# Weight slices and the first x tile of the feed-forward part: loaded from scan step 31 on, split at steps 33 to 46 in other raw places, ten slices ahead in place of nine

## The reference

```python
# attention, per head: k_n = k / (|k| + 1e-6), head_dim 48
for t in range(S):
    y[:, :, t] = q[:, :, t] @ state
    v_old = state applied to k_n[t]
    state = state + beta[t] * outer(k_n[t], v[t] - v_old)
x = y as (3072, 384)
# feed-forward 1 (d_ff 2048)
h = x @ w_in
g = (a0 + a1*h + a2*h^2 + a3*h^3) / (1 + |b0|*|h| + |b1|*h^2 + 1e-6)
x = g @ w_out
# feed-forward 2 (d_ff 2048)
x = relu(x @ w_in2)^2 @ w_out2
```

## Time and profile before

| | |
|---|---|
| time, median of 3 runs | 1114.39 us (1114.38 to 1116.54) |
| time of the profiled execution | 1114.34 us, span 1112.6 us |
| PE busy | 1094.1 us (98%) |
| DVE, ACT, POOL busy | 678.0 (61%), 650.8 (58%), 509.2 us (46%) |
| chain that ended last | PE 89%, DVE 6%, issue 2%, DMA 1%, POOL 1% |
| granted clock, mean of the span | 0.994 of 2.4 GHz |

### The profile page before, as it was taken

How to read it: one execution, slowest core, us unless ns; L and a number is a source line. 1 busy time by engine, 2 the same in 40 slices (tenths; PEclk the granted TensorE clock), 3 DMA queues, 4 the chain that set the end, 5 groups by cost and what they waited for, 6 DMA issues and landing times.

```text
span 1112.6 us, 18161 instructions
## 1 busy us (share of the span) xinstructions
PE 1094.1 (98%) x6372; PEld 944.5 (85%) x6372; DVE 678.0 (61%) x1088; ACT 650.8 (58%) x1275; POOL 509.2 (46%) x626
## 2 busy tenths in 40 slices
PE   8899999999999999999999999999999999999998
PEld 6699999999987788888888888888888888888887
DVE  6987564434559989787888879854333333434332
ACT  5566666544669777787877778653333323333322
POOL 5087888783039977887777878500000000000000
PEclk9799999999999999999999999999999999999999
DMA  8948887555531110100101002140100101010000
GB/s 193 204 84 182 165 180 151 117 94 149 135 107 57 44 57 1 32 27 1 57 1 57 1 22 93 43 128 1 57 1 9 49 1 57 0 57 1 1 29 29
DMA packets 173658, 74.41 MB, mean 67 GB/s; under 512 B 136000, under 2 KB 161728, under 8 KB 172608
## 3 DMA queue, kind: packets, MB, share of 16 engines
q1 hardware_dynamic: 163968, 68.54, 25.6%
q10 hardware_dynamic: 9600, 4.72, 1.7%
HBM read 52.27 MB, written 20.71 MB: 66 GB/s over the span
## 4 chain that ended last, share of the span: by engine, by line
PE 89%; DVE 6%; issue 2%; DMA 1%; POOL 1%; SPq 1%; ACT 0%; POOLq 0%; DVEq 0%; ACTq 0%
PE ps L1137 11%; PE ps L1139 11%; PE ps L1138 11%; PE ps L1123 11%; PE ps L1125 11%; PE ps L1124 11%; PE ps L505 3%; PE ps L484 3%; PE ps L549 3%; PE ps L535 3%; PE ps L552 3%; PE ps L515 3%; PE ps L521 2%; PE ps L467 1%; PE ps L563 1%
## 5 line engine op out<-in xcount | busy, mean ns | idle before, releaser
L1123 PE MATMUL ps<-x_split,weights 128*128 128x512 f32 x576 | 225.0, 391 | 3.8 <-DVE g_lo L1282 2.9
L1137 PE MATMUL ps<-g_hi,weights 128*128 128x512 f32 x576 | 224.1, 389 | 0.1
L1124 PE MATMUL ps<-x_split,weights 128*128 128x512 f32 x576 | 224.1, 389 | 0.0
L1125 PE MATMUL ps<-x_split,weights 128*128 128x512 f32 x576 | 224.1, 389 | 0.0
L1138 PE MATMUL ps<-g_lo,weights 128*128 128x512 f32 x576 | 224.1, 389 | 0.0
L1139 PE MATMUL ps<-g_hi,weights 128*128 128x512 f32 x576 | 224.1, 389 | 0.0
L1292 DVE TENSOR_TENSOR common<-common 128x512 f32<-128x512 f32 x96 | 66.4, 691 | 135.0 <-ACT common L1196 133.4
L1202 ACT ACTIVATE g_hi<-common 128x512 fp32r<-128x512 f32 x96 | 60.8, 633 | 141.8 <-PE ps L1139 137.3
L1123 PEld LDWEIGHTS ps<-x_split,weights 128*128 128x128 f32 x576 | 108.1, 188 | 27.9 <-DVE g_lo L1282 4.6
L1341 POOL TENSOR_SCALAR common<-common,b_abs 128x512 f32<-128x512 f32 x96 | 75.8, 789 | 116.1 <-ACT common L1171 116.1
L1355 POOL TENSOR_TENSOR common<-common,g_hi 128x512 f32<-128x512 f32 x96 | 124.4, 1296 | 9.5 <-DVE g_hi L1270 9.5
(11 more groups left out here) (121 smaller groups left out, 1917.4 us busy)
## 6 DMA issues: line engine op xcount, KB each, us to landing
scan_late<-kq_in SPq DMA_DIRECT2D x10, 768.0 KB, 5.4
scan_late<-kq_in SPq DMA_DIRECT2D x16, 384.0 KB, 4.7
shared<-w_in SPq DMA_DIRECT2D x32, 192.0 KB, 2.5
shared<-w_out SPq DMA_DIRECT2D x32, 192.0 KB, 2.6
x_first<-y_t ACTq DMA_DIRECT2D x24, 192.0 KB, 2.9
shared<-x_first SPq DMA_DIRECT2D x6, 768.0 KB, 5.8
x_second<-shared SPq DMA_DIRECT2D x6, 768.0 KB, 4.2
shared<-x_second SPq DMA_DIRECT2D x6, 768.0 KB, 5.9
```

The lines of the kernel that those rows point to most:

```text
L1123: pe.matmul(bank(n), lo, x_hi[:, slot, k, :], start=(k == 0), stop=False)
L1124: pe.matmul(bank(n), hi, x_lo[:, slot, k, :], start=False, stop=False)
L1125: mm = pe.matmul(bank(n), hi, x_hi[:, slot, k, :], start=False, stop=(k == KT - 1))
L1137: pe.matmul(ps_y[m], lo, g_hi[:, d, :], start=(f == 0), stop=False)
```

## The change

Loads and splits get tables of their own by step, and the raw places are taken in another order: slices 0 and 1 go to places 0 and 1, slices 2 and 3 to the same two places again, slices 4 and 5 to places 2 and 3, and from slice 6 on the places go round as before. A slice waits for the split of the slice that had its place (2 for 0, 3 for 1, none for 4 and 5, i-4 from 6 on).

| scan step | before: loads | before: splits | after: loads | after: splits |
|---|---|---|---|---|
| 31, 32 | | | ab and 0; 1 | |
| 33, 34 | | | x | 0; 1 |
| 35, 36 | | | 2; 3 | 2 (step 36) |
| 37 | ab, 0, x, 1, 2, 3 | | 4, 5 | 3 |
| 38 to 40 | 4, 5 (39, 40) | 0 (40) | 6, 7 (39) | x in three pieces |
| 41 to 46 | 6 to 11 | 1 to 6, x at 41, 43, 45 | 8 to 12 (42 to 46) | 4 to 9 |
| 47, 48 | 12 (47) | 7, 8 | 13 (47) | |

```diff
-    FF_LOADS, FF_SPLIT, FF_X = GROUPS - 11, GROUPS - 8, (41, 43, 45)
+    W_LOADS = {31: (0,), 32: (1,), 35: (2,), 36: (3,), 37: (4, 5), 39: (6, 7), 42: (8,), 43: (9,), 44: (10,), 45: (11,),
+               46: (12,), 47: (13,)}
+    W_SPLITS = {33: 0, 34: 1, 36: 2, 37: 3, 41: 4, 42: 5, 43: 6, 44: 7, 45: 8, 46: 9}
+    X_LOAD, X_SPLITS = 33, (38, 39, 40)
...
-                if n == FF_LOADS:
+                if n == min(W_LOADS):
                     ff.load_ab(sp)
-                    ff.load_weights(sp, 0)
+                for i in W_LOADS.get(n, ()):
+                    ff.load_weights(sp, i)
+                if n == X_LOAD:
                     ff.load_x(sp, 0)
-                    for i in range(1, ff.W_SLOTS):
-                        ff.load_weights(sp, i)
-                if 0 <= n - FF_LOADS - 2 < ff.PRE:
-                    ff.load_weights(sp, n - FF_LOADS - 2 + ff.W_SLOTS)
...
-                if 0 <= n - FF_SPLIT < ff.PRE:
-                    ff.split_weights_hi(act, n - FF_SPLIT)
+                if n in W_SPLITS:
+                    ff.split_weights_hi(act, W_SPLITS[n])
...
-    W_SLOTS, W_AHEAD, PRE = 4, 3, 9
+    W_SLOTS, W_AHEAD, PRE = 4, 3, 10
...
+    def raw_slot(i):
+        return i if i < 2 else (i + 2) % W_SLOTS
+
+    def raw_former(i):
+        return {2: 0, 3: 1}.get(i, i - W_SLOTS if i >= 6 else None)
+
+    def raw_loads(i):
+        return 1 if i < 2 else (i + 2) // W_SLOTS + (raw_slot(i) < 2)
...
-        if i >= W_SLOTS:
-            sp.wait_ge(w_lo_ready, i - W_SLOTS + 1)
+        if raw_former(i) is not None:
+            sp.wait_ge(w_lo_ready, raw_former(i) + 1)
...
-        act.wait_ge(w_loaded[i % W_SLOTS], 32 * (i // W_SLOTS) + 32)
+        act.wait_ge(w_loaded[raw_slot(i)], 32 * raw_loads(i))
```

More of the change, by code:

```diff
@@ L739, in _ @@
                     take_z_first(n)
-                if n in FF_X:
-                    ff.split_x_hi(act, FF_X.index(n), 0)
+                if n in X_SPLITS:
+                    ff.split_x_hi(act, X_SPLITS.index(n), 0)
                 spread = (n + 1 + LEAD) // 2 if n > TWICE[1] and n % 2 == 1 and end_group(n + 1) is not None else None
@@ L962, in _ @@
                         scale_v(h)
-                if n == FF_SPLIT:
+                if n == min(W_SPLITS):
                     ff.coef_bounds(dve)
[L965 to L968, removed]
+                if n in W_SPLITS:
+                    ff.split_weights_lo(dve, W_SPLITS[n])
+                if n in X_SPLITS:
+                    ff.split_x_lo(dve, X_SPLITS.index(n), 0)
             ff.vector(dve, ys_done, GROUPS)
@@ L1058, in load_weights @@
     def load_weights(sp, i):
-        m, f, slot = i // FT, i % FT, i % W_SLOTS
-        if i >= W_SLOTS:
-            sp.wait_ge(w_lo_ready, i - W_SLOTS + 1)
+        m, f, slot = i // FT, i % FT, raw_slot(i)
+        if raw_former(i) is not None:
+            sp.wait_ge(w_lo_ready, raw_former(i) + 1)
         sp.dma_start(w_raw[:, slot, 0:D_MODEL].rearrange("p (k n) -> p k n", k=KT),
@@ L1159, in split_weights_hi @@
             act.wait_ge(down_done, UNITS - FT + f + 1)
-        act.activation(weights[:, f, 0:2 * D_MODEL], w_raw[:, i % W_SLOTS], ACT.Copy).then_inc(w_hi_ready, 1)
+        act.activation(weights[:, f, 0:2 * D_MODEL], w_raw[:, raw_slot(i)], ACT.Copy).then_inc(w_hi_ready, 1)
     def split_x_hi(act, k, tile):
@@ L1246, in split_weights_lo @@
         dve.wait_ge(w_hi_ready, i + 1)
-        dve.tensor_tensor(weights[:, f, 2 * D_MODEL:4 * D_MODEL], w_raw[:, i % W_SLOTS],
+        dve.tensor_tensor(weights[:, f, 2 * D_MODEL:4 * D_MODEL], w_raw[:, raw_slot(i)],
                           weights[:, f, 0:2 * D_MODEL].bitcast(F32), ALU.subtract).then_inc(w_lo_ready, 1)
```

## The result

| | before | after |
|---|---|---|
| median, same chip, 17 runs each | 1114.68 us (1113.06 to 1117.54) | 1118.41 us (1115.89 to 1120.67) |
| ratio, 95% interval | | 1.0032 [1.0024, 1.0040] |
| span of the profiled execution | 1112.6 us | 1115.9 us |
| granted clock, mean | 0.994 | 0.992 |

The account below looks back on a forecast made before the run. PE was taken to bound the kernel, busy for 98% of the span. Gains of -2.8, a stall of +6.6 and the clock's +1.5 sum to +5.3 us: 1114.34 + 5.3 = 1119.6 us, range 1115.0 to 1122.5.

Parts of the forecast that it names:

- half clock: After the stall PE falls to 1.2 GHz for about 3.4 us: +1.5 us, bounds 0 and 3.1.
- stall before cross_z(37): ACT's split of slice 2 in step 36 waits for its loads, delaying PE's cross_z of step 37: +6.6 us.
- quad 11: Quad 11's loads go out at least a step earlier, so PE's wait around steps 43 to 45 goes: -1.0 us.
- slices 8 and 9 out of the feed-forward part: Slice 8's split leaves the first feed-forward unit, about -1.3 us; slice 9's leaves unit 6, -0.5 us.
- The hold of SP: SP is held 2.03 us on slice 2's first DMA, as on quad 10's; without it 1.5 us earlier.
- The landing: Slice 2's second DMA takes 3.7 us from its issue at 266.0, so it lands at 269.7.
- POOL's end: Splits of slices 0 and 1 delay POOL's round 5 by 1.4 us, so SP starts its store at 263.0.
- stall without the clock: Rival: the stall of 6.6 us comes but the clock does not fall: +3.8, 1118.1 us; chance 0.18.
- short wait: Rival: POOL not delayed, SP not held, slice 2 lands at 265.6, stall 2.5 us: -0.3, 1114.0 us; chance 0.12.
- no stall: Rival: ACT reaches slice 2's split only after its landing, so nothing waits: 1111.5 us; chance 0.05.
- late quad 11: Rival: slices 6 and 7 hold SP, quad 11 stays late: +1.0, 1120.6 us; chance 0.07 together with larger stall.
- larger stall: Rival: landing after 5.4 us, stall 8.3, two clock periods: +8.6, 1122.9 us; chance 0.07 together with late quad 11.

Follow-up runs that it names:

- second profile: The changed kernel run once more, unchanged: 1118.55 us, ratio 1.0027 to the kernel before.
- PE kept busy: The changed kernel with 18 added matmuls, whose results nothing reads, in front of cross_z of step 37: 1116.26 us, ratio 1.0006 to the kernel before.
- slice 2 ahead of v: The changed kernel with slice 2's loads issued between the store of round 5 and load_v(11): 1116.18 us, ratio 1.0004 to the kernel before.
- quad 11 alone: The kernel before with only slice 5's loads moved behind quad 11's, in step 41: 1114.92 us, ratio 0.9993.
- later splits: The changed kernel with slices 2 and 3 split in steps 38 and 39, not 36 and 37: 1111.10 us, ratio 0.9961 to the kernel before.
- slices 8 and 9 as before: The changed kernel with slices 2 and 3 split in steps 38 and 39, slice 8 in step 48, slice 9 at unit 6: 1114.99 us, ratio 0.9992.

## Why the prediction was right, step by step

The mechanism, the place and the sign were right. The sum was too high by 1.6 us against the runs, and by 2.0 and 2.6 against the two profiles of the changed kernel, from terms that were off both ways. In part the closeness is luck: in the first profile the stall was 2.3 us smaller than forecast and the gains 0.8 us larger, and the half clock gave 1.1 of that back. First and second profile of the changed kernel:

| term | predicted | first | second |
|---|---|---|---|
| stall before cross_z(37) | +6.6 | +4.3 | +4.8 |
| half clock | +1.5 | +2.6 | +1.5 |
| quad 11 | -1.0 | -1.0 | -1.0 |
| slices 8 and 9 out of the feed-forward part | -1.8 | -2.6 | -2.6 |
| sum | +5.3 | +3.3 | +2.7 |

(Quad 11's share is that of its own experiment; what is left of the gains is the last term.)

**The stall was the mis-sized term.** Three numbers made it up. The hold of SP, 2.03 us in the earlier trace rows, came as 2.10. The landing was 267.32 - 264.21 = 3.1 us after the issue (3.1 in the second profile and with PE kept busy too, 3.3 with slice 2 ahead of v), not 3.7: the low end of the earlier trace rows was still 0.6 too high. The third is POOL's end, forecast at 263.0 and found at 261.19. Here two things must be told apart. POOL in the changed kernel, the first instruction of round 5, the ones beside the two splits, and the last:

```profile
221.34 2.36 POOL L395 TENSOR_TENSOR shared<-shared,scan_common 128x1024 f32<-128x1024 f32 x1 [4.95 <-DMA shared<-blocks]
...
248.98 1.17 POOL L405 TENSOR_TENSOR scan_x<-shared 128x210 f32<-128x210 f32 x1
...
253.49 1.10 POOL L405 TENSOR_TENSOR scan_x<-shared 128x168 f32<-128x168 f32 x1
...
260.93 0.26 POOL L410 TENSOR_TENSOR shared<-shared,scan_x 128x30 f32<-128x30 f32 x1
```

and the round's first in the kernel before:

```profile
222.75 2.36 POOL L393 TENSOR_TENSOR shared<-shared,scan_common 128x1024 f32<-128x1024 f32 x1 [5.75 <-DMA shared<-blocks]
```

The round took 38.8 us before (222.75 to the end in the earlier trace rows) and 39.8 after; in the other seven kernels with splits in steps 33 and 34 it took 39.8 to 40.2, in the one without (quad 11 alone) 38.7. So the two splits cost POOL 1.0 to 1.3 us, against a forecast of 1.4, and the two instructions of 1.17 and 1.10 us are there. What was wrong is the start. It hangs on a load that lands when it lands, and I took the one profile of before for its place. Counted back from step 36 the round began 34.3 us ahead there, and 35.0 to 35.7 us ahead in the nine others, the kernel with quad 11 alone (35.0) among them. No edit acts before step 31, so it was an early or late start by chance, of up to 1.4 us, and in a kernel with the stall it goes whole into the stall.

With POOL's real end and 3.1 us of landing the prediction's own working gives 6.6 - 1.8 - 0.6 = 4.2 for the first profile: its steps hold, the inputs were off. The two splits do collide with POOL, by part of an instruction: the eight rounds with them are 1.0 to 1.3 us longer, and DVE's side is lengthened too (the split at 248.34 us in the first profile took 1.38 us, the next one 1.05, against 0.96 in the earlier trace rows). The rule of the Trainium skill that the prediction named ("SBUF — State Buffer", section "Who interferes with whom") gives, as an estimate with 0.96 us for each split, up to 1.9 us of POOL, and with it the stall of 7.1; the measured cost lies under that bound.

**The clock** was the uncertain choice and the value taken, 1.5 us, is one of the two that came. 2.6, 1.5 and 1.7 us (slice 2 ahead of v: 18.05 - 13.68 - 2.70) were measured for stalls of 4.3, 4.8 and 2.7 us, so the cost doesn't follow the length of the stall. It follows how long PE works at the half clock. By the grants of the stretches the half clock began 2.7 us into the idle time in the first profile, 4.3 us into it in the second, and with slice 2 ahead of v only 0.5 us after PE was at work again; that leaves 5.4, 3.1 and 3.4 us of work at 1.2 GHz (estimates from the stretches, 0.60 and 0.54 in the last), and each cost 0.48 to 0.49 of that, near the 9/20 of the prediction. Why it began where it did is open. The rival "stall without the clock" gave 1118.1, which lies nearer to the measured 1118.41 than my 1119.6, but its mechanism was wrong: the clock fell in all three profiles with such a gap. Built as the kernel with PE kept busy, it came out at a rest of +0.7 and not +3.8. Its sum had 2.3 us too much stall and 0.8 us too little gain, 3.1 us together, which by chance is about the half clock (2.6) that it left out. The statement that the clock survived 2.4 us before unit 6 did not carry over: it fell here after 2.54. Where I made the short wait decide at 5.0 us "without a fall of the clock", that condition held in none of the three profiles with such a gap.

**Quad 11** came in time, and 1.0 us is what it was worth by itself. **Slices 8 and 9** were worth 1.5 and 0.9, where 1.3 and 0.5 were taken, the second outside its bounds of 0 and 0.5. (By the medians on the one chip slice 8 is worth 2.2; the scatter ahead of step 36 is in that.) I had slice 9 remove the two short waits of 0.25 us. In fact one of them stays, and moving slice 9's split into the scan also shortens the long wait, from 1.3 to 1.0 us, though that split stood in the code at unit 6. That leaves 0.3 us of its 0.9 that no wait over 0.2 us accounts for; it is open.

**What the rivals got.** Short wait (-0.3 us against before) and no stall (-2.8) were each built: slice 2 ahead of v is the one (a rest of +0.7, since the clock went too), the later splits are the other (-3.4, and 4.9 us by the medians). The late quad 11 and the larger stall did not come.

## What to carry to other kernels

When work is moved to an earlier step, ask for each load which wait stands ahead of it in the issuing queue, and put the consumer behind the latest landing, not behind the usual one: here two steps of delay in a split turned +0.3% into -0.4%. Price a gap of PE in the middle of dense work with a loss of clock too: here it came with gaps of 2.54, 4.1 and 4.6 us, and cost 1.5 to 2.6 us. An edit that puts PE's start behind another engine's chain also takes over that engine's scatter, so read the time of that chain from more than one profile.

## What the runs showed of the hardware that was not expected

- The clock fell after idle times of 2.54, 4.1 and 4.6 us in dense work, and it then stayed at 1.2 GHz for 3.4 to 6.8 us, not the same from profile to profile: the same program lost 2.6 us once and 1.5 us once. It did not fall in a wait of 2.4 us before unit 6 (and the same with quad 11 alone and with slices 8 and 9 as before: 1.00 throughout); the 18 matmuls added in the gap kept it at 1.00.
- The last load of v (384 KB in pieces of 192 bytes) is issued in 0.4 to 0.5 us, and a DMA that follows at once on the same queue then holds SP for 2.0 to 2.1 us, whatever DMA it is (quad 10's, slice 2's, slice 3's). An earlier one, directly behind quad loads, took 2.02 us itself. What in SP or the queue takes that time is not shown.
- Landing of a raw slice took 3.1 us behind the store and v and 3.3 us behind the store alone, under the smallest (3.7) that the kernel before had shown from 240 to 284 us and over its median of the whole run (2.6).
